# Loading the second expert layer and the last matrix with neighbouring rows in one partition

## What is computed

```python
# attention: batch 4, heads 8, sequence 768, head size 64; 8 global keys, 96 local ones
a = softmax(scale * q @ k.T + bias, masked);  x = a @ v          # x: 3072 x 512
# soft mixture of experts: 8 experts with 4 slots each
logits = x @ phi                                                 # 3072 x 32
slot_input = softmax(logits over tokens).T @ x                   # 32 x 512
for e in range(8):
    h = relu(slot_input[e] @ w1[e])                              # w1: 512 x 1024
    slot_out[e] = h @ w2[e]                                      # w2: 1024 x 512
x = softmax(logits over slots) @ slot_out
# last network
g = relu(x @ w_in) ** 2;  out = g @ w_out                        # w_in 512 x 2048, w_out 2048 x 512
```

## Time and profile before

| what | value |
|---|---|
| median of 3 runs | 514.47 us (513.95 to 515.8) |
| profiled execution, its own time | 514.65 us |
| its span | 512.9 us |
| granted TensorE clock, mean | 0.993 |
| PE busy | 488.4 us, 95% |
| DVE, ACT, POOL busy | 363.5, 346.5, 94.8 us |
| moved by DMA | 77.24 MB in 24,587 packets |

### The profile page before, as it was taken

One profiled execution on the slowest core, in us unless ns is written; L12 is line 12 of the kernel. 1 busy time (PEld: TensorE's weight loads), 2 busy tenths in 40 slices (PEclk: granted clock), 3 DMA queues, 4 the chain that ended last, 5 costly groups with the idle time before them and its releaser, 6 DMA issues.

```text
span 512.9 us, 12775 instructions
## 1 busy us (share of the span) xinstructions
PE 488.4 (95%) x4573; PEld 399.3 (78%) x4573; DVE 363.5 (71%) x1024; ACT 346.5 (68%) x758; POOL 94.8 (18%) x223
## 2 busy tenths in 40 slices
PE   2999999999999998689999999999999999999997
PEld 1767766776666642324789999999999999999996
DVE  6687786787787671305998987787776877858783
ACT  2788887887888610005998977777677777777740
POOL 1455544545445303400000000000000000000000
PEclk9999999999999999799999999999999999999999
DMA  7699889884565699996001011010100101011011
GB/s 288 242 359 360 332 300 326 327 320 140 177 199 173 210 346 411 385 386 245 0 1 43 0 43 42 1 41 0 41 21 20 41 0 41 0 41 41 0 42 42
DMA packets 24587, 77.24 MB, mean 151 GB/s; under 512 B 2400, under 2 KB 2400, under 8 KB 22112
## 3 DMA queue, kind: packets, MB, share of 16 engines
q1 hardware_dynamic: 19536, 60.95, 32.7%
q10 hardware_dynamic: 5008, 15.73, 8.3%
HBM read 70.39 MB, written 6.29 MB: 150 GB/s over the span
## 4 chain that ended last, share of the span: by engine, by line
PE 83%; DVE 6%; ACT 4%; issue 2%; POOL 2%; DMA 1%; ACTq 0%; DVEq 0%; POOLq 0%
PE bank L1551 14%; PE bank L1552 14%; PE bank L1553 14%; PE bank L1232 7%; PE bank L1220 4%; PE bank L1523 4%; PE bank L1247 4%; ACT probs L974 3%; PE bank L1457 3%; PE bank L1477 3%; PE bank L1252 2%; PE bank L1282 2%; POOL probs L435 2%; PE bank L1272 2%; PE bank L1215 2%
## 5 line engine op out<-in xcount | busy, mean ns | idle before, releaser
L974 ACT ACTIVATE probs<-probs,nmax 128x232 f32<-128x232 f32 (+1 forms) x192 | 88.6, 463 | 33.4 <-DVE nmax L525 33.4
L435 POOL TENSOR_SCALAR probs<-probs,rden 128x232 f32<-128x232 f32 (+1 forms) x192 | 82.8, 452 | 91.9 <-DVE rden L534 91.9
L1551 PE MATMUL bank<-t_hi,s_hi 128*128 128x256 f32 x352 | 98.7, 280 | 0.0
L1552 PE MATMUL bank<-t_lo,s_hi 128*128 128x256 f32 x352 | 98.6, 280 | 0.0
L1553 PE MATMUL bank<-t_hi,s_lo 128*128 128x256 f32 x352 | 98.5, 280 | 0.0
L525 DVE CUSTOM_DVE_ANT_0 probs<-bank,bias 128x232 f32<-128x232 f32 (+1 forms) x192 | 61.7, 378 | 25.2 <-PE bank L1220 21.8
L1097 ACT ACTIVATE g_s<-bank 128x1024 f32<-128x1024 f32 x48 | 49.0, 1023 | 30.5 <-PE bank L1523 30.5
L1126 ACT ACTIVATE s_hi<-s 128x512 fp32r<-128x512 f32 x88 | 55.1, 627 | 19.1 <-DVE s L908 14.6
L1551 PEld LDWEIGHTS bank<-t_hi,s_hi 128*128 128x128 f32 x352 | 66.5, 189 | 0.0
L1552 PEld LDWEIGHTS bank<-t_lo,s_hi 128*128 128x128 f32 x352 | 66.4, 189 | 0.0
L1553 PEld LDWEIGHTS bank<-t_hi,s_lo 128*128 128x128 f32 x352 | 66.4, 189 | 0.0
(11 more groups left out here) (189 smaller groups left out, 997.0 us busy)
## 6 DMA issues: line engine op xcount, KB each, us to landing
qkv_s<-qkv_dram SPq DMA_DIRECT2D x15, 1028.0 KB, 7.5
qkv_s<-qkv_dram SPq DMA_DIRECT2D x16, 704.0 KB, 5.0
w_s<-w_dram ACTq DMA_DIRECT2D x5, 2048.0 KB, 9.7
w_s<-w_dram SPq DMA_DIRECT2D x15, 512.0 KB, 8.6
out_dram<-o_stage SPq DMA_DIRECT2D x24, 256.0 KB, 2.0
w_a<-w_dram SPq DMA_DIRECT2D x9, 512.0 KB, 8.2
wo_raw<-w_out_dram SPq DMA_DIRECT2D x4, 1024.0 KB, 13.4
w_pre<-w_dram ACTq DMA_DIRECT2D x1, 2048.0 KB, 13.0
```

The lines of the kernel that those rows point to most:

```text
L435: last = pool.tensor_scalar(probs[:, v % 2, m, a, 0:w], probs[:, v % 2, m, a, 0:w], rden[:, v % 2, m, a:a + 1], 1.0, ALU.mult, ALU.mult)
L974: act.activation(probs[:, v % 2, m, a, 0:w], probs[:, v % 2, m, a, 0:w], ACT.Exp, bias=nmax[:, v % 2, m, a:a + 1], scale=-1.0, accum_out=d ...
L1551: pe.matmul(OUT[n], hi, W_HI[n](at_f), start=(c == 0 and f == 0 and n in (0, 2, 4, 5)), stop=False, skip_group_check=True)
L1552: pe.matmul(OUT[n], hi, W_LO[n](at_f), start=False, stop=False, skip_group_check=True)
```

## The change

The two views become `(p c)`: partition p holds the rows 8p to 8p+7 of an expert's second-layer matrix (block c is row 8p + c), and the rows 16p to 16p+15 of `w_out`. A partition's shares of neighbouring blocks are then neighbours in memory. Because block f now stands for the rows f, f+8, f+16, ..., the transposes of `h_s` read every eighth column from f on, and mix reads the columns of `w_in` in the order f, f+16, f+32, ... for each block f, so that block f of `mix` again fits block f of `w_out`. The number, order and size of all instructions and loads stay as they are.

```diff
-        w2_v = w2.rearrange("e (c p) n -> e p c n", p=P)
+        w2_v = w2.rearrange("e (p c) n -> e p c n", p=P)
@@ block.sync
-                sp.dma_start(wo_raw[:, blocks, :], w_out.rearrange("(c p) n -> p c n", p=P)[:, blocks, :]).then_inc(wo_in[n], 16)
+                sp.dma_start(wo_raw[:, blocks, :], w_out.rearrange("(p c) n -> p c n", p=P)[:, blocks, :]).then_inc(wo_in[n], 16)
@@ block.tensor, transposes of h_s
-                    last = pe.transpose(bank[2 + f // 4][:, (f % 4) * P:(f % 4 + 1) * P], h_s[:, f * P:(f + 1) * P], ident[:, :])
+                    last = pe.transpose(bank[2 + f // 4][:, (f % 4) * P:(f % 4 + 1) * P], h_s[:, bass.ds(f, P, step=FEC)], ident[:, :])
@@ block.tensor, mix
-                    last = pe.matmul(bank[0][SLOTS * n:SLOTS * (n + 1), :], so_t[:, c, :], win[:, n * 512:(n + 1) * 512],
+                    last = pe.matmul(bank[0][SLOTS * n:SLOTS * (n + 1), :], so_t[:, c, :],
+                                     win.rearrange("p (q f) -> p f q", f=FFC)[:, GF * n:GF * n + GF, :],
                                      start=(c == 0), stop=(c == DC - 1), tile_position=(0, SLOTS * n))
```

## The result

The changed kernel takes 517.98 us (median of 8 runs, 517.15 to 519.68), the kernel before, run beside it, 514.33 us (8 runs, 513.44 to 516.13). The ratio is 1.0071, with a 95% interval of 1.0059 to 1.0084: slower by 3.0 to 4.3 us. The forecast was 517.5 us. The profiled execution took 518.05 us with a span of 516.3 us, 3.4 us more span than before.

A forecast was written before the change was run, and what follows sets the result against it. The bound was taken to be the chain of waits through the expert layers, transposes and mix, not the loads. 514.65 us + 0 (loads) + 1.1 (transposes) + 2.0 (mix) = 517.7, given as 517.5 us; range 513.6 to 525.0 us.

The forecast's parts named there:

- The two terms: Strided reads on the chain: +2.0 us in mix and +1.1 us in the transposes of both expert groups.
- DVE's ratio of 1.58: Price of DVE's strided SBUF read against contiguous, applied to PE: 0.58 x 3.43 = 2.0 us for mix.
- the lower bound of that step: Transposes of `h_s`: 0 us, if the stationary load (141 ns, overlapped) has time to spare.
- the sign that was named for the transposes: L1464 on the chain: eight transposes over 1.6 us instead of 1.08, with stationary loads above 141 ns.
- Rival 1: Mix and transposes: PE's fp32 passes leave the read ports time, strided reads are free; 514.5 us; chance 0.30.
- Rival 2: Mix's four side-by-side streams hinder each other at a shared port: +6.9 to +10.3 us, 522 to 526.5 in all; chance 0.20.
- Half speed for every separate read: PE at half speed in both places: mix +3.4 us, transposes +1.8 us, in all 519.9 us.
- The loads at no cost: Loads of `w2` and `w_out`: up to 2 us less transfer from longer runs, effect on the end 0.
- Their room: Last part of `w2` through at about 228 us, needed by PE at 231.86 us: 3.6 us of room.
- Rival 3: Second expert group: the clock dip from 210 to 212 us vanishes, saving 2.5 us, 512.0 us with free strided reads; chance 0.05.

The follow-up runs named there:

- `idle_far`: The kernel before, but the fp32r filler matmuls read their moving columns 16 bytes apart: 516.64 us in one execution.
- the exchanged loops: The kernel before with mix's two loops exchanged: 519.29 us with neighbouring columns, 526.92 us with the changed kernel's strided columns, one execution each.
- `loads_only`: The kernel before with both (p c) views, transposes and mix reading neighbouring columns as before: 514.45 us against 514.34, ratio 1.0004.
- `before_no4`: The kernel before without the four filler matmuls in the second group's second layer: 513.83 us, ratio 0.9994.
- `experts_only`: The kernel before with only the (p c) view of `w2` and the strided transposes: 514.34 us against 514.34, ratio 0.9999.
- the last four runs: Kernel before without four fillers, 0.9994; same with `w2` joined and transposes strided, 0.9978; all loads joined, mix reading neighbouring columns, with fillers 1.0000, without 0.9975.

## Why the prediction was right, point by point

- **Direction, size and place** were right: 517.5 us forecast, 517.98 measured, all of it in reading `w_in` and `h_s` at a distance. That the size came out so close is partly luck, as the next point shows.
- **The two terms were each off, in opposite directions.** Mix was put at +2.0 us and measured +3.40. The step that failed is taking DVE's ratio of 1.58 for PE, which the prediction itself called a thin basis: PE's is 2.0 for a moving operand (0.43 to 0.86 us a round). The transposes were put at +1.1 us for both groups and measured +0.14. There the stationary load did pay a ratio (141 to 194 ns, 1.38), but it is not what sets their pace; the lower bound of that step, named and not taken, was nearly the truth, and the sign that was named for the transposes (over 1.6 us instead of 1.08) did not come: they took 1.15. The sum of 3.1 us stands against 3.4 us in the spans and 3.65 in the medians.
- **Rival 1** (hidden) had argued with fp32's slow 0.84 ns a column. That leaves no time: fp32 and fp32r streams are both halved. **Rival 2** (shared port) fell with `idle_far` and the lone records of the exchanged loops.
- **Half speed for every separate read**, the size that the prediction put beside the rule of the Trainium skill (Advanced Engine Details and Errata, Memory Cachelines), which gives none, made +3.4 us for mix, and that came; for the transposes it made 1.8 us, of which 0.14 came.
- **The loads at no cost** held for this change (`loads_only`, 1.0004). Their room was overrated, though. I worked out from bytes that the last part of `w2` is through at about 228 us, 3.6 us ahead of PE; `before_no4` shows PE waiting for it until 230.56 us, and `experts_only` until 230.65, so the room was about 1.3 us. The rows of before gave it away: the first two parts of `w_out` land at 233.01 and 235.64 us, 2.6 us apart, so the load before them lands at about 230.4.
- **Rival 3** (the clock) was overpriced at 2.5 us. In the profiled execution of `experts_only` the dip was missing and the time hardly better, because a PE that is ahead there meets the loads of `w2`, and one that comes more than 0.76 us sooner to the end of mix hands the chain to ACT and `w_out`. The dip changes between executions of one kernel, and with it most of their spread: of the 35 executions of the kernel before that stand beside the last four runs, the 14 with a mean clock of 0.995 or more took 513.3 to 514.2 us, the 18 at 0.992 to 0.993 514.1 to 515.5, and the 3 at 0.990 516.0 to 516.3. From the middle to the first group that is 0.9 us in the medians, not 2.5. No edit here was shown to bring the dip or to take it away.

## What to carry to other kernels

When a layout is changed so that loads get longer runs, ask who pays for the distance. Here it was moved from loads that the chain did not wait for to the moving operand of a matmul on the chain, where floats 16 and 64 bytes apart halve the pace; put in a read of PSUM by ACT or DVE it cost nothing. And a load that no engine waits for is worth nothing sooner, until something in front of it is shortened: here the two had to come together (0.41 us without the fillers alone, not clear of none; about 1 us with joined rows as well).

## What the runs showed of the hardware that was not expected

- A matmul's moving operand read from SBUF: floats 8 bytes apart cost some 5% (a round of 0.45 us against 0.43), 16 and 64 bytes apart 2.0 to 2.1 times: in fp32 with four streams side by side (0.43 to 0.86 us at 64 bytes), in fp32 with one alone in its column group (the same two paces), and in fp32r with one over the whole array at 16 bytes (0.23 to 0.46 us).
- A stationary operand of 128 floats 32 bytes apart loads in 194 ns instead of 141, and eight transposes get slower by no more than 0.07 us.
- ACT and DVE read PSUM 16 bytes apart at full pace (0.61 and 0.70 us for 128x512), while DVE's reduction from SBUF at 128 bytes had shown 1.58 times a contiguous one.
- With the loops exchanged, matmuls of the same column group followed each other every 0.43 us a record, no faster than a round of four groups side by side; those of the next group began while four of the eight records of the group before were still to come, so that 16 matmuls took 8.88 us where 13.7 was expected.
